# One low-part tile of the MLP input moves from GpSimd to VectorE, and a wait on the query leaves GpSimd's program

## The reference

```python
scores = scale * q @ k.T ; causal mask ; a = softmax(scores)
local = a @ v
mem_out = (phi(q) @ M_prev) / (phi(q) @ z_prev + 1e-6)       # phi(x) = elu(x) + 1
x = g * mem_out + (1 - g) * local                            # [2304, 512]
x = (sigmoid(x @ w_gate) * (x @ w_val)) @ moe_w_out          # d_ff 1536
h = x @ w_in
return (h * clip(h + 3, 0, 6) / 6) @ moe2_w_out              # d_ff 2048
```

## Time and profile before

| | us |
|---|---|
| median of 3 runs | 1068.94 |
| lowest to highest | 1068.53 to 1069.87 |
| profiled execution, its own time | 1068.94 |
| its span | 1067.1 |
| PE busy | 1045.1 |
| DVE busy | 711.9 |
| ACT busy | 638.1 |
| POOL busy | 537.3 |

### The profile page before, as it was taken

The page is one execution under the profiler, slowest core; times in us unless marked ns, Lnnn a source line. Parts: engine busy times, 40 slices in busy tenths (PEclk is TensorE's granted clock), DMA queues, the critical chain, the costliest instruction groups (busy, mean ns, idle before and its releaser), DMA issues.

```text
span 1067.1 us, 20596 instructions
## 1 busy us (share of the span) xinstructions
PE 1045.1 (98%) x6740; PEld 984.0 (92%) x6740; DVE 711.9 (67%) x1540; ACT 638.1 (60%) x1436; POOL 537.3 (50%) x563
## 2 busy tenths in 40 slices
PE   5999999999999999999999999999999999999998
PEld 4778999999999999999999999989988888888997
DVE  5997777877877877877745444766676655665553
ACT  5887776777777777776755433465556334543333
POOL 5997567569667669667536654158880101000000
PEclk9999999999999999999999999999999999999999
DMA  8553443442543442542223244354555443454411
GB/s 193 137 141 76 115 112 89 120 115 79 132 116 87 117 120 73 133 119 78 72 68 109 90 136 153 103 176 164 173 184 175 123 117 119 119 172 120 121 52 60
DMA packets 126348, 126.90 MB, mean 119 GB/s; under 512 B 12080, under 2 KB 92464, under 8 KB 126000
## 3 DMA queue, kind: packets, MB, share of 16 engines
q1 hardware_dynamic: 125968, 122.07, 39.8%
q10 hardware_dynamic: 288, 3.67, 0.9%
HBM read 106.30 MB, written 19.40 MB: 118 GB/s over the span
## 4 chain that ended last, share of the span: by engine, by line
PE 95%; DVE 3%; issue 1%; ACT 1%; DMA 0%; SPq 0%; DVEq 0%; ACTq 0%
PE ps L817 89%; PE ps L858 5%; PE ps L871 1%; DVE prob L1571 1%; DMA qk_st<-qk_t 0%; DVE q_s L1479 0%; DVE phi L1552 0%; DVE Cb L1768 0%; DVE znorm_e L1542 0%; DVE znorm L1540 0%; DVE x_lo L1599 0%; DVE raw L1772 0%; DVE phi L1536 0%; DVE rsum_e L1524 0%; ACT raw L1377 0%
## 5 line engine op out<-in xcount | busy, mean ns | idle before, releaser
L817 PE MATMUL ps<-x_hi,WG 128*128 128x288 f32 x1536 | 322.0, 296 | 0.0
L817 PEld LDWEIGHTS ps<-x_hi,WG 128*128 128x128 f32 x1536 | 250.7, 188 | 0.6
L817 PE MATMUL ps<-x_lo,WG 128*128 128x288 f32 x768 | 226.1, 294 | 0.0
L817 PE MATMUL ps<-XC,WC 128*128 128x384 f32 x1008 | 202.5, 336 | 2.1 <-DVE Cb L1768 1.7
L817 PEld LDWEIGHTS ps<-XC,WC 128*128 128x128 f32 x1008 | 180.3, 188 | 17.6 <-issue 3.2
L672 POOL TENSOR_TENSOR WG<-stage,WG 128x512 fp32r<-128x512 f32 x96 | 124.4, 1315 | 95.5 <-ACT WG L1188 95.4
L817 PE MATMUL ps<-wo,G_hi 128*128 128x512 f32 x540 | 168.0, 392 | 0.0
L817 PE MATMUL ps<-h_hi,WO 128*128 128x288 f32 x768 | 164.6, 297 | 0.2 <-DVE Y L1741 0.2
L817 PEld LDWEIGHTS ps<-x_lo,WG 128*128 128x128 f32 x768 | 144.3, 188 | 0.5
L1768 DVE TENSOR_TENSOR Cb<-ps,Cb 128x384 f32<-128x384 f32 x168 | 89.1, 554 | 83.2 <-PE ps L817 81.4
L702 POOL TENSOR_SCALAR prob<-prob,rscale 128x128 f32<-128x128 f32 (+4 forms) x160 | 103.6, 666 | 73.3 <-DVE rscale L1530 73.3
(11 more groups left out here) (137 smaller groups left out, 1990.7 us busy)
## 6 DMA issues: line engine op xcount, KB each, us to landing
WC<-w_in_parts SPq DMA_DIRECT2D x112, 256.0 KB, 2.7
stage<-w_out SPq DMA_DIRECT2D x64, 256.0 KB, 2.7
qk_st<-qk_t SPq DMA_DIRECT2D x54, 288.0 KB, 4.2
stage<-w_gate SPq DMA_DIRECT2D x48, 256.0 KB, 3.3
stage<-w_val SPq DMA_DIRECT2D x48, 256.0 KB, 2.9
w_in_parts<-WC SPq DMA_DIRECT2D x42, 256.0 KB, 2.0
qn_st<-q_n SPq DMA_DIRECT2D x16, 256.0 KB, 3.3
w_in_parts<-WC ACTq DMA_DIRECT2D x2, 1792.0 KB, 7.0
```

Of the source, the lines that this page charges most:

```text
L817: return pe.matmul(o, l, r, start=start, stop=stop, skip_group_check=True)
```

## The change

Tile 0 of `x_lo` is no longer written by POOL in `middle_x`, but by DVE in slot 2 of step p = 1, between O3's addition and `low_q`. POOL keeps tiles 1 and 2, and no longer waits for `q_ready` before them. The semaphores `xc_lo` and `xc_lo_mid` count 2 and 2 tiles of a batch, where they counted 1 and 3.

```diff
         HIGH_X = {1: (0,), 2: (1, 2), 3: (3,)}
-        LOW_X = {4: (3,)}
-        MIDDLE_X, OUTER_X = (0, 1, 2), (3,)
+        LOW_X = {2: (0,), 4: (3,)}
+        MIDDLE_X, OUTER_X = (1, 2), (0, 3)
...
-            def middle_x(n, b):
-                if not is_last(n, 1):
-                    pool.wait_ge(q_ready, 2 * (n + 1) + 1)
+            def middle_x(b):
                 for k in MIDDLE_X:
                     pool.wait_ge(xc_hi, DT * b + k + 1)
                     pool.tensor_tensor(x_lo[:, k, :], x_new[:, k, :], x_hi[:, k, :].bitcast(F32), ALU.subtract).then_inc(xc_lo_mid, 1)
...
-            def low_ws(n, r, p, cut, alone):
+            def low_ws(r, p, cut, alone):
...
                     if cut is not None and p == 1 and i == 2:
-                        middle_x(n, cut)
+                        middle_x(cut)
...
-                low_ws(n, r, p, cut, not (scoring or old))
+                low_ws(r, p, cut, not (scoring or old))
```

## The result

The changed kernel takes 1076.41 us (median of 6 runs, 1075.95 to 1077.21) against 1068.74: ratio 1.0069, 95% interval 1.0059 to 1.0081. It is slower by 7.4 us in spans (1074.5 against 1067.1) and by 7.7 in the medians.

A forecast was written before the change was run, and what follows sets the result against it. PE, busy 98% of the span, was taken to bound the kernel. Two waits of 2.7 us, less about 0.1 for overlapping starts, add 5.3 us to 1068.94: 1074.2 us, range 1071.3 to 1076.2.

The forecast's parts named there:

- PE's wait at O6: First two cuts: tile 0 and `low_q` held by POOL delay O4's addition, so O6 starts 2.7 us late in each.
- Who is first: At DVE's tile 0 in the first two cuts: POOL starts its tile 0.09 us earlier, so DVE is held.
- one hold-up: Rival: in each cut only DVE's tile 0 or `low_q` is held; 1.43 us per cut, 1071.8 us; chance 0.17.
- The removed wait costs nothing: POOL's wait on `q_ready`, 0.94 us idle before its three tiles, is off PE's path; removing it gains 0.
- Gain on the path: 0: POOL's lost subtraction and lost wait on `q_ready` are both off PE's path, so removing them gains 0.
- each of the two cuts is worth 2.7 us in full: O6's delay in each of the first two cuts counts fully, since PE has no idle time to win it back.
- A second wait: Rival: at tile 3, ACT's delay and the clash with `low_w` reach G0; up to 1 us more per cut, 1076.2; chance 0.07.
- Third cut, 0: Third cut: DVE's tile 0 moves O4's addition by 0.05 us and PE by nothing.
- Faster: Rival: POOL freed early lets DVE's tile 3 fall from 1.89 to 0.76 us; at most 3.4 us gained, 1065.5; chance 0.03.

The follow-up runs named there:

- wait_back: Changed kernel with POOL's wait on `q_ready` before its own tiles put back, tile 0 staying on DVE: ratio 0.9999 to the kernel before, cut pairs 40.39 us.
- wait_only_gone: Kernel before with only POOL's wait on `q_ready` taken away, all three middle tiles staying on POOL: ratio 1.0012, cut pairs 40.98 and 41.00 us.
- query_late: Changed kernel with `low_q` moved behind O5's addition in the pairs with a cut: ratio 1.0010 to the kernel before, cut pairs 40.88 and 40.87 us.
- slot3_wait: Changed kernel with POOL's wait on `q_ready` put back and DVE's tile 0 one slot later, behind O5's addition: ratio 1.0007 to the kernel before.
- repaired: Changed kernel with POOL waiting for DVE's tile 0 before its own tiles, and `low_q` behind O5's addition in cut pairs: ratio 1.0002 to the kernel before.
- first_cut_only: Kernel before with the change made in the first cut alone: ratio 1.0045, cut pairs 44.36 and 40.17 us.
- shifted: Changed kernel with two more 128x576 DVE subtractions ahead of the first key's low part: ratio 1.0096 to the kernel before, cut pairs 44.22 and 42.88 us.
- slot3_quiet: slot3_wait with POOL held back from slot 3's two weight blocks until DVE has written tile 3: ratio 1.0015 to the kernel before, cut pairs 40.65 us.

## Why the prediction was right, and where it was off

The forecast was 1074.2 us, slower; measured were 1076.41, 0.2 above the top of the range. Of the 7.7 us between the medians the two pairs account for 6.9; the rest lies before them and isn't shown to be the change's. By its steps:

- *PE's wait at O6, 2.7 us in each of two cuts.* Right: 2.61 in the first and 2.62 in the second. The steps behind it held too: POOL first, tile 0 held (1.9 us forecast, 2.06 measured), POOL's tile 2 in between, `low_q` held (2.0 forecast from 249.37 to 251.39, 1.86 measured). wait_back, wait_only_gone and query_late each took one part away and lost about what that part was priced at. The Trainium skill's rule (SBUF — State Buffer, section Who interferes with whom) is borne out in each of these traces: 0.75 us alone, about 2 us when POOL is ahead. That POOL's waiting instruction comes before DVE's next, taken from the earlier trace rows, was right in both cuts.
- *Who is first.* Right, but by less than was thought. The forecast gave POOL a lead of 0.09 us. Measured it was at most 0.01: both engines started at 247.80 in the first cut, POOL at 411.22 and DVE at 411.23 in the second, because DVE's tile 0 started before the addition ahead of it was over. The chance of the other order (one hold-up, 1071.8) was larger than the rows seemed to say, and some luck is in this step.
- *The removed wait costs nothing.* The prediction put the wait down under "Gain on the path: 0" and counted its absence through the hold-ups, where POOL is first because nothing keeps it. That was right in the sum, but only half of the matter: the wait alone was worth 0.8 us for each pair (wait_only_gone).
- *The term that was missing* is PE's clock. I took a wait of 2.6 us at its own length. One of the two is followed by 3 us at 0.50, which costs another 1.5. With it the sum is 2 x 2.6 + 1.5 + 0.1 for the next point = 6.8, and the pairs say 6.88. Here the step "each of the two cuts is worth 2.7 us in full" failed; why one wait is hit and the other not stays open: it doesn't go with the place in the kernel.
- *A second wait.* I put the next narrow point at tile 3 of `x_lo`, with a cover of 0.9 us. It is the low part of head tile 3, which stands behind tile 3 and O7 in DVE's queue and which G1 waits for. In the changed kernel it cost about 0.1 us in the first cut (2.73 - 2.61), so the sum hardly suffered, but slot3_wait and repaired missed their expectations by 0.31 and 0.17 us for each pair through it.
- *Third cut, 0.* Right. DVE's tile 0 took 0.85 us there, and the next addition started right behind it, without a wait of PE:

```profile
572.82 0.85 DVE L1584 TENSOR_TENSOR x_lo<-x_new,x_hi 128x576 fp32r<-128x576 f32 x1
573.64 0.46 DVE L1739 TENSOR_TENSOR Y<-ps,Y 128x288 f32<-128x288 f32 x1
```

- *Faster.* Not borne out by repaired and wait_back: with the hold-ups gone the pairs are 0.17 and 0.22 us longer than in the kernel before, not shorter, since PE has no idle time in those pairs for POOL's work to give back.

In first_cut_only, shifted, repaired and slot3_quiet the pair after the second cut, which has no cut, was 0.2 to 0.4 us longer, in first_cut_only although the second cut was left as it is in the kernel before. I haven't followed that up.

## What to carry to other kernels

When an engine is saturated, look at a change on the others for what it puts ahead of the instruction that frees the saturated engine's next bank, and measure the cover there (0.5 us here), not the engine's busy share. A wait between two engines that seems to serve no data can be what keeps their instructions from stopping each other: before taking it away, lay the two timelines side by side and ask who starts first, and don't trust a lead of a tenth of a microsecond that is worked out from rounded ends. And a stall of PE may have to be priced above its own length: here 2.4 us cost 1.5 more in four of six places, while the stalls of 0.45 and 0.34 us left the clock alone.

## What the runs showed of the hardware

A wait of PE of 2.3 to 2.4 us after steady work was followed by about 3 us at a granted clock of 0.50 (1.2 GHz) at four of six places in four profiles. In two of these kernels, equal but for two more subtractions at the start, the place that was hit changed from the second cut to the first. When a subtraction of DVE with two SBUF inputs met one of POOL, the one that started 0.01 to 0.14 us earlier went first and the other stood until it was over: where POOL was first, DVE's ended about 0.6 us after POOL's. When both kept coming back to back, they took turns (POOL's tile 1, DVE's tile 0, POOL's tile 2, DVE's `low_q`, in both cuts of the changed kernel).
